# A linear-attention and two-layer kernel: the state increment product is issued ahead of the three output products

## The reference

```
for t in range(S):                       # attention: 4 batches, 8 heads, 768 positions, 48 wide
    state = alpha[t][:, None] * state + outer(k[t], v[t])
    y[t] = q[t] @ state
x = y as 3072 tokens of 384
h = x @ w_in;  x = (h * cos(h)) @ w_out                      # block 1, 384 -> 2048 -> 384
h = max(x @ w1, x @ w2, x @ w3);  out = h @ w_out            # block 2, 384 -> 768 -> 384
```

## Time and profile before

| | us |
|---|---|
| median of 3 runs | 840.66 (840.27 to 841.2) |
| the profiled execution | 840.65 |
| its span, first to last instruction | 839.0 |
| PE busy in the span | 822.1 (98%) |
| PEld busy | 756.6 (90%) |
| DVE, ACT, POOL busy | 579.0, 427.8, 246.5 |
| mean granted clock of PE | 0.998 of full speed |

### The profile page before, as it was taken

The page is one execution under the profiler, slowest core; times in us unless marked ns, Lnnn a source line. Parts: engine busy times, 40 slices in busy tenths (PEclk is TensorE's granted clock), DMA queues, the critical chain, the costliest instruction groups (busy, mean ns, idle before and its releaser), DMA issues.

```text
span 839.0 us, 15508 instructions
## 1 busy us (share of the span) xinstructions
PE 822.1 (98%) x5446; PEld 756.6 (90%) x5446; DVE 579.0 (69%) x1078; ACT 427.8 (51%) x933; POOL 246.5 (29%) x270
## 2 busy tenths in 40 slices
PE   5899999999999999999999999999999999999998
PEld 5899998888888888888888888899999999999997
DVE  7887867777777768776875577677565655665554
ACT  5887775444554444445444466554343434344333
POOL 7986763434344424441542133200000000000000
PEclk9999999999999999999999999999999999999999
DMA  9833333222232204220321001210111110100001
GB/s 285 244 95 86 88 86 96 58 58 57 55 99 57 58 29 124 58 58 29 95 82 61 34 24 57 95 57 1 39 39 38 39 38 37 37 37 0 1 39 38
DMA packets 14034, 54.68 MB, mean 65 GB/s; under 512 B 1952, under 2 KB 2464, under 8 KB 13968
## 3 DMA queue, kind: packets, MB, share of 16 engines
q1 hardware_dynamic: 13248, 49.90, 20.5%
q0 software_dynamic: 720, 3.93, 1.2%
HBM read 44.39 MB, written 9.44 MB: 64 GB/s over the span
## 4 chain that ended last, share of the span: by engine, by line
PE 92%; POOL 3%; ACT 2%; issue 2%; DVE 1%; DMA 0%; ACTq 0%; POOLq 0%; DVEq 0%
PE h_ps L1297 7%; PE h_ps L1299 6%; PE h_ps L1298 6%; PE acc_pair L1297 5%; PE acc_pair L1298 5%; PE acc_pair L1299 5%; PE h_ps L1403 4%; PE score L1403 4%; PE h_ps L1405 4%; PE h_ps L1404 4%; PE score L1405 4%; PE score L1404 4%; PE acc_last L1297 3%; PE acc_last L1299 3%; PE acc_last L1298 3%; PE score L1261 2%
## 5 line engine op out<-in xcount | busy, mean ns | idle before, releaser
L458 POOL TENSOR_TENSOR work<-work 128x512 f32<-128x512 f32 (+1 forms) x90 | 119.4, 1327 | 278.2 <-DVE work L995 261.6
L638 ACT ACTIVATE work<-work 128x512 f32<-128x512 f32 (+1 forms) x112 | 63.7, 569 | 134.7 <-POOL work L458 122.9
L1297 PE MATMUL h_ps<-x_hi,w_hi 128*128 128x512 f32 (+1 forms) x282 | 110.9, 393 | 2.3 <-POOL w_lo L448 1.8
L981 DVE TENSOR_TENSOR work<-work,h_ps 128x512 f32<-128x512 f32 (+1 forms) x94 | 58.5, 622 | 67.1 <-ACT work L638 66.6
L1299 PE MATMUL h_ps<-x_lo,w_hi 128*128 128x512 f32 (+1 forms) x282 | 104.0, 369 | 0.0
L1298 PE MATMUL h_ps<-x_hi,w_lo 128*128 128x512 f32 (+1 forms) x282 | 103.3, 366 | 0.0
L873 DVE RECIPROCAL inv_decay<-decay 112x128 f32<-112x128 f32 x96 | 89.6, 941 | 0.5
L645 ACT ACTIVATE g_hi<-work 128x512 fp32r<-128x512 f32 (+1 forms) x112 | 63.4, 566 | 42.7 <-DVE work L981 41.4
L1297 PE MATMUL acc_pair<-g_hi,w_hi 128*128 128x512 f32 (+1 forms) x224 | 81.9, 366 | 0.5 <-POOL g_lo L466 0.3
L1298 PE MATMUL acc_pair<-g_hi,w_lo 128*128 128x512 f32 (+1 forms) x224 | 80.4, 359 | 0.0
L1299 PE MATMUL acc_pair<-g_lo,w_hi 128*128 128x512 f32 (+1 forms) x224 | 80.4, 359 | 0.0
(11 more groups left out here) (229 smaller groups left out, 2397.8 us busy)
## 6 DMA issues: line engine op xcount, KB each, us to landing
v_all<-val SPq DMA_DIRECT2D x24, 576.0 KB, 3.7
raw<-qka SPq DMA_DIRECT2D x44, 291.0 KB, 4.7
block_out<-x SPq DMA_DIRECT2D x6, 768.0 KB, 5.9
x_in<-block_out SPq DMA_DIRECT2D x6, 768.0 KB, 4.2
raw<-wb SPq DMA_DIRECT2D x12, 384.0 KB, 3.1
out<-raw POOLq DMA_DIRECT2D x5, 768.0 KB, 3.5
stage_own<-wa SPq DMA_DIRECT2D x6, 384.0 KB, 7.0
x<-wa SPq DMA_DIRECT2D x6, 384.0 KB, 5.4
```

The source lines that it names most:

```text
L458: nc.gpsimd.tensor_tensor(frac[:, cols], turns[:, cols], whole[:, cols], ALU.subtract).then_inc(S["frac_done"], 1)
L638: nc.scalar.activation(cosine[:, cols], frac[:, cols], ACT.Sin, scale=-TURN if half and t < POOL_FRAC else TURN).then_inc(S["cos_done"], 1)
L981: nc.vector.tensor_tensor(gated[:, cols], cosine[:, cols], h, ALU.mult).then_inc(S["g_done"], 1)
L1297: mm(ps, w_hi[:, w_at], xh, start=first, stop=False, skip_group_check=shared)
```

## The change

In the steps with attention `increment` of a unit is called before `outputs` of the same unit. Two producers that reuse what both read, `load_v` on SP and `mul_decay` on POOL, wait for `y_done` beside `inc_done`, with the same count. The first increment of a pair waits for the pair's `v_all` itself. The opening phase keeps its order.

```diff
--- before.py
+++ after.py
@@ -301,6 +301,7 @@
 
             def load_v(a, p):
                 wait(sp, "inc_done", BATCH * (PAIRS * a + p - 1))
+                wait(sp, "y_done", BATCH * (PAIRS * a + p - 1))
                 sp.dma_start(v_all[:, p % 2], val[a, p]).then_inc(S[f"v_in{p % 2}"], 16)
 
             def load_weights(k):
@@ -430,6 +431,7 @@
                 s, g = p % 2, 4 * a + p
                 pool.wait_ge(S["scan_done"], g + 1)
                 wait(pool, "inc_done", BATCH * (g - 1))
+                wait(pool, "y_done", BATCH * (g - 1))
                 mul(q_dec[R, s, :, hi], raw_qk[R, s, 0, :, hi], decay[R, s, :, D_HI], ALU.mult)
                 return mul(k_dec[R, s, :, lo], raw_qk[R, s, 1, :, lo], decay[R, s, :, D_LO], ALU.mult)
 
@@ -1288,6 +1290,8 @@
                 pe.wait_ge(S["mask_done"], n + 1)
                 if n < FIRST_UNITS:
                     wait(pe, "state_done", 2 * (n + 1 - depth))
+                if b == 0 and n >= UNITS:
+                    pe.wait_ge(S[f"v_in{p % 2}"], 16 * (2 * a + p // 2 + 1))
                 mm(ps, scores[:, s, KEYS_AT], v_all[:, p % 2, b, 0], start=True,
                    stop=True).then_inc(S["inc_done"], 1)
 
@@ -1466,8 +1470,8 @@
                     if attend:
                         if i < last:
                             stage1(c + 1, i + 1)
+                        increment(c + 1, i)
                         outputs(c + 1, i)
-                        increment(c + 1, i)
                 if lag == 3:
                     accumulate(last - 2)
                 accumulate(last - 1)
```

## The result

| us | before | after |
|---|---|---|
| median of 8 runs | 840.94 (840.26 to 841.88) | 838.41 (837.83 to 838.98) |
| ratio after / before, 95% | | 0.997 (0.9961 to 0.9979) |
| the profiled execution | 840.65 | 838.1 |
| its span | 839.0 | 836.4 |

The changed kernel is faster by 0.3%, and the interval leaves out both no change and the 0.2% that I had called the bound of what can be told. Forecast were 839.0 and a range of 838.0 to 840.9: the time lies in the range, and the gain is 2.5 us where I had counted 1.64.

The account below looks back on a forecast made before the run. PE, busy 98% of the span, was taken to bound the kernel. Half step 0.48 plus full steps 1.34 less 0.18 gave -1.64 us, so 840.65 became 839.0; range 838.0 to 840.9 with rivals, 838.5 to 839.6 without.

Parts of the forecast that it names:

- rival 1: Gain comes whole, as PE's waits before unit 4's scores and for g_lo move with PE: 838.2 to 838.5; chance 0.13.
- That PE's own stream decides: PE, busy 98% of the span: only what shortens or lengthens its stream, or makes it wait, can move the time.
- The small products, 0.028 us a unit: Each attention unit's small products on PE: reordered loads hide better, 0.028 us less a unit, bounds 0 and 0.04.
- the same tile product behind them: Large products behind each unit's small ones: taken as the same in both kernels, so no term was given to them.
- The reading of rows 3: PE's weight loads in one unit: load-to-load distance is the larger of this pass's load and the stream before it.
- What the waits give back: PE's waits rooted elsewhere eat earlier units' gains: three units in each of four full steps, one unit at each step's end.
- The hole at 86 us: Half step, fifth unit: increment fills 0.20 of PE's 0.34 us hole, so -0.20 there instead of -0.14.
- The last unit, +0.18: Last unit of c = 4: y_done comes about 0.18 us later, so PE's wait for g_lo grows by 0.18.
- The other edits at nothing: Later x_high, added y_done and v_in waits, earlier inc_done: nothing; at most 0.05 each for 20 if v_in needs an instruction.
- Rival 2: The order is worth nothing on PE; the half step's -0.20 and last step's +0.18 leave 840.65; chance 0.14.
- Rival 3: Tile product's load behind L1280's 112-row product cannot be hidden: slower, up to +6.4 us, 847.0, if wholly exposed; chance 0.08.

Follow-up runs that it names:

- waits_only: The changed kernel with outputs again called before increment, so only the added waits remain, against the kernel before: 840.9 against 841.26 us, ratio 0.9997.
- wide_last: Old order, outputs first, with the increment product moving 128 columns instead of 96, against the kernel before: 840.48 against 841.26 us, ratio 0.9995.

## Why the prediction was right, and where it was off

The sign, the mechanism and the places of the waits held; one term, the gain of a unit, was mis-sized, too small in the full steps and too large in the half step. That the time still fell into the range is in part luck: the gain of a full unit, 47 ns, is outside the bounds that I gave it (0 to 0.04 us), and the range reached far enough down only because of rival 1, whose mechanism did not hold.

- **That PE's own stream decides:** right. `waits_only` is the kernel before; the order alone makes the gain.
- **The small products, 0.028 us a unit:** the part that I worked out measured 24 ns. From the load of the first product behind the transpose's to that of the tile's second product it is 921 ns before and 897 after, with L1297's load hidden, and the output's first load behind the increment showing 85 ns, as read from rows 3. In the rows of the kernel after, above: 184.44 to 184.55 is again 0.11 for the tile's first load.
- **The step that failed is the sentence ahead of it,** that both kernels run "the same tile product behind them", at the same speed. In a full step the tile product is 23 ns shorter as well, in the half step 10 longer. So the term is 0.047 in full steps and 0.013 in the half step. My upper bound of 0.04 was too low, because it was built from the small products' spacings alone; rows 3 ended with the second load of the tile, where the wide spacings begin (185.04 to 185.27).
- **The reading of rows 3,** that a distance is the larger of this pass's own load and the stream before it, holds for the passes that move, but not for every pass. In the kernel before, just ahead of rows 3:

```profile
183.84 0.30 PEld L1262 LDWEIGHTS score<-q_dec,k_split 112*128 112x128 f32 x2
184.01 0.20 PEld L1263 LDWEIGHTS score<-ident,k_dec 112*128 112x128 f32 x1
```

Two loads of 128 columns take 0.17 here (110 and 58 ns), where the reading has 0.11 for each. It is the same after, and so no part of the difference; why this load doesn't show is open.
- **What the waits give back:** right in place and nearly in size. Before unit 4's scores 0.39 (forecast 0.36); with 47 instead of 28 ns a unit it had to be more. Of a full step's 16 units 12 count: 12 x 47 ns = 0.56, measured 0.55. The wait that I took to be at the end of the other steps too is there: at the end of c = 1 the last distance before tile 15's accumulate is 258 ns before and 321 after, the gain of about one unit.
- **The hole at 86 us:** right. It was to fall under 0.2. The row after, beside the earlier trace rows:

```profile
86.20 0.20 PEld L1265 LDWEIGHTS score<-ident,k_dec 112*128 112x128 f32 x1
86.31 0.28 PEld L1295 LDWEIGHTS score<-v_all,scores 128*112 128x112 f32 x2
86.68 0.24 PEld L1278 LDWEIGHTS y_ps<-scores,v_all 128*96 128x96 f32 x2
```

The increment's two passes of 0.10 run from 86.31; the next load could follow at 86.51 and comes at 86.68, so 0.17 of the hole is left.
- **The last unit, +0.18:** measured 0.19 by undoing it, 0.15 in the stretch. PE's wait there is 0.47, forecast 0.4.
- **The other edits at nothing:** right (`waits_only`).
- **The sum with the measured sizes:** half step 0.20 + 10 x 0.013 = 0.33 (measured 0.36 without unit 0's waits), full steps 4 x 12 x 0.047 = 2.26, less 0.18: 2.41, where the attention stretch lost 2.43. With 0.028 it was 1.64.
- **The rivals.** The time lies among those of rival 1 (838.2 to 838.5), but its mechanism fell: the waits did not move with PE, the one before unit 4 grew by 0.11 and took 0.49 us in all. Rival 2 fell with the rhythm, and with it the rule that the prediction took from the Trainium skill, page "TensorE: Matmul & The Clock Gate", section "The mechanism", that a load overlaps a running matmul only when its row group differs. In `wide_last` too, loads of 112 and 128 columns vanish behind 128-column streams. The prediction left out that the same section also names the background weight buffer as a case in which a load is pulled ahead, which would fit what is seen here. Rival 3 fell: L1301's load behind the product of 112 rows shows no more than L1297's did.

## What to carry to other kernels

When a kernel is bound by PE, the distances between weight loads give the price of an order: put a wide load behind a long stream, and a short stream ahead of a narrow load. But read the rhythm over a whole unit, the large products behind the small ones included, and not just over the passes that move; a bound built from the moved passes alone (0.04) did not hold what came (0.047). And before counting units, find the wait in each stage whose root does not move with PE: it keeps what the units ahead of it gain (0.49 of 2.92 us here), and one edit on the other engine (here two calls swapped on DVE) gives it back.

## What the runs showed of the hardware

- Large products that follow small fp32 ones, or a wait of PE, do not start at their steady speed. With 512 columns they came at mostly 228 to 236 ns for one to ten products and at 227 from then on, at a granted clock of 1.00; behind small products the length of this stretch changed with their order and widths and cost 4 to 56 ns a unit. What sets it is open.
- The distance from unit to unit was a whole number of steps of 6.67 ns in every kernel (810, 811, 813 or 815, 817 steps in full steps, 517, 519, 521 or 522 in the half step).
- A wait costs less than its idle time: 0.39 us idle before unit 4's scores cost 0.21.
- In the full steps a small product could be lengthened at nearly no cost: 64 more moving columns in two passes cost 7 ns in the new order and saved 20 in the old one. In the half step they cost 33 and 17.
- The Trainium skill, page "TensorE: Matmul & The Clock Gate", section "LDWEIGHTS (loading the stationary operand)", gives a load as its columns / 1.2 in ns, so 80, 93 and 107 for 96, 112 and 128. Where loads showed here they took 81 to 87, 98 to 99 and 110 to 112 ns between starts: the trace agrees to within 7 ns.
